# Where the gates' table is turned: after the first gather in the feed-forward block, or in the expert block around the first row turn

## The reference, cut to what matters

```
logits = xn @ en.T / tau                      # 3072 x 8
expert_idx = np.argmax(logits, axis=1)
probs = np.exp(logits - logits.max(-1, keepdims=True))
probs /= probs.sum(-1, keepdims=True) + 1e-09
gate_w = probs[np.arange(N), expert_idx]      # one gate per token
for e in range(E):
    mask = expert_idx == e
    h = np.maximum(x[mask] @ w1[e], 0.0)      # 384 -> 1024
    out[mask] = gate_w[mask, None] * (h @ w2[e])   # 1024 -> 384
```

## Time and profile before

| | us |
|---|---|
| median of 3 runs (lowest, highest) | 913.72 (911.74, 915.76) |
| the profiled execution | 913.93 |
| its span, first to last record | 912.2 |
| attention block and feed-forward block up to the last feed-forward product | 0 to 569.7 |
| routing and the start of the expert block, up to the first expert product | 569.7 to 603.75 |
| the expert tiles | 603.75 to the end |

### The profile page before, as it was taken

The page is one execution under the profiler, slowest core; times in us unless marked ns, Lnnn a source line. Parts: engine busy times, 40 slices in busy tenths (PEclk is TensorE's granted clock), DMA queues, the critical chain, the costliest instruction groups (busy, mean ns, idle before and its releaser), DMA issues. The chain is left out here.

```text
span 912.2 us, 18540 instructions
## 1 busy us (share of the span) xinstructions
PE 858.1 (94%) x5068; PEld 766.4 (84%) x5069; DVE 600.2 (66%) x960; ACT 474.3 (52%) x1213; POOL 332.5 (36%) x373
## 2 busy tenths in 40 slices
PE   4888888999999999999999999889999999999995
PEld 4677776888899899899899898779899899998995
DVE  9899995899999999999999997711211112112110
ACT  3444445666777777777777766222333333323331
POOL 8577774222333433434334332112222222322211
PEclk8799999999999999999999999789999999999998
DMA  8689894211686886886886797378836846811100
GB/s 224 200 247 280 254 263 123 89 44 53 209 278 222 268 275 222 274 271 216 279 271 209 261 313 249 114 294 312 310 127 231 317 141 218 308 41 34 50 4 1
DMA packets 109177, 184.59 MB, mean 202 GB/s; under 512 B 11371, under 2 KB 35085, under 8 KB 109136
## 3 DMA queue, kind: packets, MB, share of 16 engines
q1 hardware_dynamic: 95184, 168.54, 56.6%
q0 software_dynamic: 3968, 10.82, 3.6%
q10 hardware_dynamic: 9984, 4.72, 1.9%
HBM read 119.55 MB, written 65.86 MB: 203 GB/s over the span
## 5 line engine op out<-in xcount | busy, mean ns | idle before, releaser
L1088 POOL TENSOR_TENSOR ew_l<-ew_raw,ew_h 128x512 fp32r<-128x512 f32 x96 | 126.5, 1325 | 213.3 <-DVE poly L1282 213.3
L1005 PE MATMUL y_ps<-wout_h,g_h 128*128 128x392 f32 x384 | 132.0, 344 | 4.1 <-ACT x_sb L1196 3.1
L1006 PE MATMUL y_ps<-wout_l,g_h 128*128 128x392 f32 x384 | 130.6, 340 | 0.0
L1007 PE MATMUL y_ps<-wout_h,g_l 128*128 128x392 f32 x384 | 130.4, 340 | 0.0
L1428 DVE TENSOR_TENSOR ex_hT_l<-e_bank,ex_hT_h 128x512 fp32r<-128x512 f32 x62 | 39.9, 686 | 125.1 <-ACT ex_hT_h L1572 125.1
L1005 PE MATMUL h_ps<-xT_h,win 128*128 (+1 forms) x288 | 113.1, 393 | 1.6 <-DVE diff L1263 1.6
L1006 PE MATMUL h_ps<-xT_l,win 128*128 (+1 forms) x288 | 112.7, 391 | 0.0
L1007 PE MATMUL h_ps<-xT_h,win 128*128 (+1 forms) x288 | 112.4, 390 | 0.0
L1455 POOL DMA_INDIRECT out_dram<-ex_o_sb,put_i x31 | 31.0, 1001 | 209.4 <-ACT ex_o_sb L1556 209.4
L1176 ACT ACTIVATE g_h<-poly 128x512 fp32r<-128x512 f32 x96 | 61.1, 637 | 85.5 <-DVE poly L1282 85.0
L1420 DVE TENSOR_TENSOR ex_xT_l<-e_bank,ex_xT_h 128x384 fp32r<-128x384 f32 x31 | 17.3, 558 | 123.0 <-ACT ex_xT_h L1548 108.2
(11 more groups left out here) (192 smaller groups left out, 1988.0 us busy)
## 6 DMA issues: line engine op xcount, KB each, us to landing
ew_raw<-in_w SPq DMA_DIRECT2D x96, 256.0 KB, 3.1
w_h<-ew_h SPq DMA_DIRECT2D x96, 256.0 KB, 3.2
w_l<-ew_l SPq DMA_DIRECT2D x96, 256.0 KB, 2.3
w_ex<-w_h SPq DMA_DIRECT2D x14, 1536.0 KB, 6.9
w_ex<-w_l SPq DMA_DIRECT2D x14, 1536.0 KB, 11.6
rT_sb<-in_rT SPq DMA_DIRECT2D x48, 96.0 KB, 3.1
kT_sb<-in_kT SPq DMA_DIRECT2D x48, 96.0 KB, 3.2
k_sb<-in_k SPq DMA_DIRECT2D x24, 192.0 KB, 3.3
```

The lines of the kernel that those rows point to most:

```text
L1005: pe.matmul(out, lh, rh, start=start, stop=False)
L1006: pe.matmul(out, lh, rl, start=False, stop=False)
L1007: return pe.matmul(out, ll, rh, start=False, stop=stop)
L1088: pool.tensor_tensor(ew_l[:, slot, :], raw, ew_h[:, slot, :].bitcast(F32), ALU.subtract).then_inc(ew_l_made, 1)
```

## The change

It does five things.

1. The feed-forward block ends with the first gather. The gathers of tiles 1 and 2 move to the head of POOL's work in the expert block.
2. The gates' table pass moves to the expert block: `rhs_gate` is made there by DVE, in four operations of half the width instead of two, and PE turns 12 of the 24 columns before the first row turn and 12 after it. The result is taken by DVE after the first tile's split, and POOL waits for it (`gates_made`) before it copies the first gate.
3. `expert_at` and `ends_at` are made earlier, between the last step of the exponential's input and the wait for the first pass.
4. `keep_warm` of 4 between the passes, of 16 at the start of the expert block and of 4 after the first turn go; one of 4 stands at the start of the expert block. In rows of the trace, that is 8 where there were 48.
5. SP begins with expert 1's weights only when PE has turned all gates. `ex`, `gates` and `gate_l` lie in the buffer `quad` instead of `ew_raw`.

```
         def route_gpsimd(pool):
             pool.wait_ge(x2_stored, 16 * NT)
             pool.wait_ge(rows_found, 1)
-            for i in range(FETCH):
-                pool.indirect_dma_start(rows_sb[:, i * DM:(i + 1) * DM], None, x2_dram, ...
+            pool.indirect_dma_start(rows_sb[:, 0:DM], None, x2_dram, ...
...
             last.then_inc(ids_turned, 1)
-            keep_warm(pe, h_ps[1], ident, 4)
-            pe.wait_ge(gates_placed, 2)
-            for n in range(NT):
-                last = pe.matmul(gate_ps, oh_slot[:, n, :], rhs_gate[:, n, :, :].rearrange("p a s -> p (a s)"),
-                                 start=(n == 0), stop=(n == NT - 1))
-            last.then_inc(gates_turned, 1)
...
             @block.sync
+                sp.wait_ge(gates_turned, 1)
                 sp.wait_ge(gathered[FETCH - 1], 16)
...
+                def place_gates():
+                    for at in range(0, NT, PART):
+                        for part, x in ((0, gate_h[:, at:at + PART].bitcast(F32)), (1, gate_l[:, at:at + PART])):
+                            dve.tensor_tensor(rhs_gate[:, at:at + PART, part, :], in_tile[:, at:at + PART, :],
+                                              x.unsqueeze(2).to_broadcast([P, PART, COLS]),
+                                              ALU.mult).then_inc(gates_placed, 1)
+                def take_gates():
+                    dve.wait_ge(gates_turned, 1)
+                    dve.tensor_copy(gate_high[:, :], gate_ps[:, 0:ST]).then_inc(g_step, 1)
+                    dve.wait_ge(g_step, 1)
+                    dve.tensor_tensor(gate[:, :], gate_high[:, :], gate_ps[:, COLS:COLS + ST],
+                                      ALU.add).then_inc(gates_made, 1)
+                place_gates()
                 x_low(0, 0, 0)
+                take_gates()
                 loop(dve, tile)
...
+                for i in range(1, FETCH):
+                    pool.indirect_dma_start(xg[:, i, :], None, x2_dram, ...
+                pool.wait_ge(gates_made, 1)
                 gate_of(0, 0, 0)
...
-                keep_warm(pe, banks[7], ident, 16)
+                def turn_gates(first):
+                    pe.wait_ge(gates_placed, 2 * (first // PART + 1))
+                    for n in range(first, first + PART):
+                        last = pe.matmul(gate_ps, oh_slot[:, n, :], rhs_gate[:, n, :, :].rearrange("p a s -> p (a s)"),
+                                         start=(n == 0), stop=(n == NT - 1))
+                    return last
                 pe.sem_inc(tile_done, 1)
+                keep_warm(pe, y_ps[1], ident, 4)
+                turn_gates(0)
                 transpose_tokens(0, 0, 0)
-                keep_warm(pe, banks[7], ident, 4)
+                turn_gates(PART).then_inc(gates_turned, 1)
                 loop(pe, tile)
```

More of the change, by code:

```diff
@@ L132, in build @@
                       ident, consts, rtau, win_h, win_l, w_logit)
-            feed_forward(nc, x2_dram, xg_sb, load_group, xg_loaded, xt_stored, ident, consts, win, w_ex, w_out, w_logit,
-                         sumsq, w12, w12_h, w12_l, rows_sb, get_row, put_row, gate, expert_at, ends_at, gathered,
+            placed = feed_forward(nc, x2_dram, xg_sb, load_group, xg_loaded, xt_stored, ident, consts, win, w_ex, w_out, w_logit,
+                         sumsq, w12, w12_h, w12_l, rows_sb, get_row, put_row, expert_at, ends_at, gathered,
                          first_loaded)
         experts(nc, x2_dram, out, w_ex, w12_h, w12_l, ident, rows_sb, get_row, put_row, gate, expert_at, ends_at, gathered,
-                first_loaded)
+                first_loaded, *placed)
 def attention(nc, rT, kT, r, k, v, w, u_row, w_in, w_outT, emb, tau, x_dram, load_group, x_sb, x_stored,
@@ L784, in feed_forward @@
         below = part_of(spare, [P, NT, E])
-        ex = part_of(spare, [P, NT, E])
+        ex = part_of(spare_q, [P, NT, E])
         norm = part_of(spare, [P, 4, NT])
@@ L793, in feed_forward @@
         slot = part_of(spare, [P, NT])
-        gates = part_of(spare, [P, 2, NT])
-        gate_l = part_of(spare, [P, NT])
+        gates = part_of(spare_q, [P, 2, NT])
+        gate_l = part_of(spare_q, [P, NT])
         table = part_of(spare, [P, ST])
@@ L830, in route_gpsimd @@
             pool.wait_ge(rows_found, 1)
-            for i in range(FETCH):
-                pool.indirect_dma_start(rows_sb[:, i * DM:(i + 1) * DM], None, x2_dram,
-                                        bass.IndirectOffsetOnAxis(ap=get_row[:, i:i + 1],
-                                                                  axis=0)).then_inc(gathered[i], 16)
+            pool.indirect_dma_start(rows_sb[:, 0:DM], None, x2_dram,
+                                    bass.IndirectOffsetOnAxis(ap=get_row[:, 0:1], axis=0)).then_inc(gathered[0], 16)
         def route_scalar(act):
@@ L927, in route_vector @@
             dve.tensor_tensor(below[:, :, :], below[:, :, :], wide(norm[:, 2, :], E), ALU.mult).then_inc(shifted, 1)
+            step(dve.tensor_tensor(passed[:, :, :],
+                                   tile_ids[0:1, 0:ST].unsqueeze(2).to_broadcast([1, ST, E - 1]),
+                                   tend[0:1, 0:E - 1].unsqueeze(1).to_broadcast([1, ST, E - 1]), ALU.is_ge))
+            step(dve.tensor_reduce(empty[0:1, :], passed[:, :, :], AX.X, ALU.add))
+            dve.tensor_copy(expert_at[:, :], empty[0:1, :]).then_inc(r_dve, 1)
+            dve.tensor_copy(ends_at[:, :], tend[0:1, :]).then_inc(r_dve, 1)
+            done[0] += 2
             dve.wait_ge(ids_turned, 1)
@@ L941, in route_vector @@
             step(dve.tensor_tensor(gate_l[:, :], gates[:, 1, :], gate_h[:, :].bitcast(F32), ALU.subtract))
[L942 to L955, removed]
         SPLIT = [9, 11, 13]
@@ L1465, in tile @@
                         gate_of(*later(i, j, k, 1))
+                for i in range(1, FETCH):
+                    pool.indirect_dma_start(xg[:, i, :], None, x2_dram,
+                                            bass.IndirectOffsetOnAxis(ap=get_row[:, i:i + 1],
+                                                                      axis=0)).then_inc(gathered[i], 16)
+                pool.wait_ge(gates_made, 1)
                 gate_of(0, 0, 0)
```

14 lines of the change are left out of this document (10 added, 4 removed).

## The result

| | before | after |
|---|---|---|
| median of 20 runs (lowest, highest), us | 915.0 (911.74, 917.39) | 911.07 (907.4, 914.12) |
| the profiled execution; its span, us | 913.93; 912.2 | 908.92; 907.1 |
| first expert product, us after `get_row` starts | 19.40 | 12.44 |
| end of the span, us after `get_row` starts | 327.85 | 323.08 |

A forecast was written before the change was run, and what follows sets the result against it. Bound taken: the routing chain from `get_row` to the first expert product. That product 8.45 us earlier, less 2.2 for the low clock, gives 6.25 us: 913.93 becomes 907.7, the median 907.5 us (range 905.0 to 910.2).

The forecast's parts named there:

- The barrier: Between feed-forward and expert block: POOL done at 586.75, 0.43 us taken as before, so PE begins at 587.2.
- rival C: At the block's end POOL is held until its gather lands: PE begins at 589.2, gain 4.2 us, 909.5; chance 0.12.
- The base: The starting time: a median of 913.72 us, 0.2 below the profiled execution's 913.93.
- PE's part of the block: Expert block: empties 2.06 us, gates' products 2.67 twice, turn 0.6, number's load 0.1; first expert product at 595.3.
- The number's load: Ahead of tile 0's first expert product: loading the expert number is hidden behind twelve products, 0.1 us instead of 1.06.
- rival B: Ahead of the first expert product the number's load stays unhidden, 1.06 us: gain 5.2, time 908.5; chance 0.2.
- The clock: In tile 0 the clock starts at 0.50 and rises after 4.8 us (3.5 to 6.5), a loss of 2.2 us.
- A: The clock rises at or before the first expert product: gain about 8.4 us, time 905.3; chance 0.08.
- D: The clock stays low through the first tiles: loss from 18 us on, 919 at 30 us; chance 0.04.
- The edits at no cost: Ahead of `get_row`: the earlier `expert_at` and `ends_at` delay it by 0.1 us, at most 0.3.
- The sum's cover: Ahead of `get_row`: DVE's wait of 1.16 us for PE's first pass, just used up by the moved operations.

The follow-up runs named there:

- e5: The kernel after with all three gathers back at the end of the feed-forward block; ratio 0.9975 to the kernel before.
- f1: e1 plus one 64 KB plain DMA issued by POOL after `get_row`, awaited by nobody; ratio 0.9926 to the kernel before.
- e1: The kernel after with the first gather too moved to the head of POOL's work in the expert block; ratio 0.9921 to the kernel before.
- f2: e1 plus one 768 KB DMA issued by SP after `get_row`, awaited by nobody; ratio 0.9916 to the kernel before.
- d1: The kernel before with the change's fewer empty products alone (8 rows instead of 48); ratio 0.9966 to the kernel before.
- e2: e1 plus two unused 128x512 subtractions by POOL at the end of the feed-forward block; ratio 0.9935 to the kernel before.
- h1: e1 plus 5 more empty products behind the routing's first pass, ahead of the barrier; ratio 0.9932 to the kernel before.
- e3: The kernel after with 16 empty products (32 rows) at the start of the expert block instead of 4; ratio 0.9949 to the kernel before.
- e4: e1 without any empty products at the start of the expert block; ratio 0.9919 to the kernel before.
- g3: e4 with gates' products split: 12 ahead of the turn, 6 behind it, 6 behind tile 0's first half; ratio 0.9922 to the kernel before.

## Why the prediction was wrong

**The barrier, the step that failed.** "I take the same when POOL is last: PE begins at 587.2", 2.85 us after `get_row`, measured 5.06: 2.21 us more. That was rival C, "the barrier holds POOL until its gather has landed", with a chance of 0.12 and a time of 909.5. C's place for PE, +4.85, and its gain, 4.2 us, are both close (+5.06; 3.9 by the medians, 4.77 in the profiled pair). Against it I had said that no wait on the gather stands at the block's end in the order. That is true and was no evidence: the order shows the program's own waits, and this one is not among them. The kernel after, e5 and f1 show PE's start 0.6 to 0.7 us behind the landing, e1 and f2 a start that nothing holds where no DMA of POOL is in flight. What in POOL waits, no run here shows. Taking C's chance low was also a fault of reading: no barrier of this trace had been reached with a POOL DMA in flight, so the 0.43 us came from a row of another kind. They were short even for a barrier without a DMA, which took 0.82 us in e1 and 0.83 in f2. My estimate from these: POOL's issue ended at +2.30, and +3.1 would have been PE's start without the hold, so 1.9 of the 2.21 us are the hold and 0.3 the barrier itself.

**The base.** The forecast leaned on three runs with a median of 913.72; twenty have 915.0. That is 1.3 us, the second reason why the time lies outside the range. Either alone would have left it inside: 915.0 less the predicted 6.25 is 908.75, and 907.5 with 2.2 more for the barrier is 909.7. With both, 915.0 less C's 4.2 is 910.8, against a measured 911.07.

**PE's part of the block.** Predicted 8.1 us from the first empty row to the first expert product, measured 7.38: 8 rows in 1.70 us from start to start (2.06 taken, which is the duration with its tail), twelve gates' products 2.56 twice (2.67), the turn 0.56 (0.6), nothing at the end (0.1). So the first product came 1.49 us later than forecast: +2.21 and -0.72.

**The number's load (rival B).** No idle time of "issue" stands ahead of the product at 596.46. Hidden, as forecast; the 1.06 us of the earlier trace rows are part of the gain. (B's own sum took off the whole 1.06 us though 0.1 of it was already in: it should read 5.3 us and 908.4.)

**The clock (rivals A and D).** Predicted a rise 4.8 us after the first product and a loss of 2.2 us in tile 0. Measured: 5.0 us, and 6.56 us (596.46 to 603.02) for the first half of tile 0 where 4.33 would do at the full clock (before's from 603.75 on), so 2.23. The 512-column products stand (600.87 - 597.03) / 9 = 0.427 us apart at the low clock; the Trainium skill (TensorE: Matmul & The Clock Gate, "Back-to-back issue gap") puts the gap of N columns at that clock at about N / 1.2 ns, which is 427 ns for 512, and the trace agrees. The size of the loss is in part chance. In before, after, d1, e1, e2, f1 and h1 the clock stayed low for 17.1 us in all (584.4 to 601.5 after the change), so it rose the sooner behind the first expert product the longer before it it had fallen. It was low for a shorter time in e3, e4, f2 and g3 and for a longer one in e5.

**The edits at no cost.** The extra DVE operations did delay `get_row`, by about 0.5 us instead of the 0.1 (at most 0.3) of the sum, though it starts earlier (584.02 against 584.35). PE's first pass starts at 580.02 before and at 580.00 after; it takes 4.07 us (580.02 to 584.09) before, where the clock fell at 582.1 in the middle of it (0.53 in 582 to 583, then 0.50), and 3.24 us after, where it fell at 584.4 (1.00 until 584, 0.71 in 584 to 585). The sum's cover, DVE's wait of 1.16 us, rested on the slow pass. In the kernel after DVE could have copied at 583.24 and copied at 583.82, behind its own work; in d1, with a pass of 3.24 us too and without the moved operations, DVE waits 0.34 us and copies 0.04 us behind the pass. The length of the pass is not due to the edit: e2 has the code of after up to there, and its pass took 4.07 us.

SP loads expert 1 from 596.67 and the next from 617.08; tile 3 starts at 624.22, and between 603 and 900 the view of waits has for PE only the two of before:

```profile
PE e_bank L1495 <- ACT ex_o_sb L1576: 1.3, 1, 1.3
PE e_bank L1495 <- DVE ex_xT_l L1411: 0.5, 1, 0.5
```

**The account.** First product 19.40 - 12.44 = 6.96 us sooner, less 2.23 for the clock, is 4.73, and the end comes 4.77 sooner. With 0.33 from the earlier `get_row` this is the 5.1 us between the two spans. Counted from the end of PE's first pass instead, which leaves in what the moved operations cost, the end comes 328.11 - 323.86 = 4.25 us sooner, and the other 0.85 us are the shorter pass, luck of the two profiled executions. The medians say 3.9, with both 4.25 and 4.77 inside their interval.

## What to carry to other kernels

Before a block's end is moved forward, look for DMAs that POOL has issued in it: in these traces the block lasted until they had landed, some 3 us for a gather, though the program waited for nothing. Issue them behind the barrier if they are not wanted at once; here that alone brought the change from 0.9956 to 0.9921, a kernel (e1) that beats both; the intervals of e2, e4, f1, f2, g3 and h1 overlap with its own. Empty products that only warm the clock are to be weighed whole: 24 more rows cost 4.4 us and gave it all back, and three runs of a kernel can stand 1.3 us beside its median.

## What was not expected of the hardware

- The end of the block waited for POOL's DMAs in flight (gathers of 3.3 and 2.9 us, a plain copy of 2.0), and not for SP's (3.2).
- Beside POOL's two 128x512 subtractions (e2) two of DVE's 128x24 operations took 0.74 and 0.85 us instead of 0.18, while the one between them kept its 0.30. One trace shows it; that sharing is the cause is argued.
- Gates' products of 64 columns take 0.213 us each at the low clock and 0.113 at the full one. They never raised it: 0.50 all through the earlier trace rows, the kernel after and h1, where 32 rows of empties did (e3, at 593.1, 4.1 us after the first).
- The clock came back between 3.1 and 5.9 us after the first expert product, in kernels whose tile 0 is the same. The first half of tile 0 then took 5.70 us in e4 and 6.89 in f1. This is over 1 us of difference that no edit explains, and e4's lead over e1 is mostly that. The plainest pair is e1 and f2: PE's instructions are the same and the first product comes at +10.07 and +10.06, yet the clock rose 5.6 us behind it in e1 and 4.1 in f2.
